# A fused attention and mixture kernel: w_in compacted in three spans of columns, and w2's last half summed in banks of its own

## The reference, cut to what matters

```python
attn_out = softmax(scale * q @ k.T + bias, causal window of 128) @ v        # 4 batches, 8 heads, 576 tokens, 64
x = attn_out as (2304, 512)

logits = x @ phi                                   # (2304, 32): 8 experts with 4 slots each
slot_input = softmax(logits, over tokens).T @ x    # (32, 512)
for e in range(8):                                 # w1[e]: 512 x 1024, w2[e]: 1024 x 512
    slot_out[e] = maximum(slot_input[e] @ w1[e], 0) @ w2[e]
c = softmax(logits, over slots)                    # (2304, 32)
x = c @ slot_out                                   # (2304, 512)

h = x @ w_in                                       # w_in: 512 x 2048
g = h * clip(h + 3, 0, 6) / 6
out = g @ w_out                                    # w_out: 2048 x 512
```

## Time and profile before

| | |
|---|---|
| median of 3 runs | 426.57 us (426.09 to 427.25) |
| the profiled execution | 426.3 us, span 424.5 us |
| TensorE matmuls busy | 415.3 us (98%) |
| VectorE busy | 234.5 us (55%) |
| ScalarE busy | 215.5 us (51%) |
| GpSimd busy | 70.6 us (17%) |
| DMA | 61.36 MB, mean 145 GB/s |

### The profile page before, as it was taken

One profiled execution on the slowest core, in us unless ns is written; L12 is line 12 of the kernel. 1 busy time (PEld: TensorE's weight loads), 2 busy tenths in 40 slices (PEclk: granted clock), 3 DMA queues, 4 the chain that ended last, 5 costly groups with the idle time before them and its releaser, 6 DMA issues.

```text
span 424.5 us, 9722 instructions
## 1 busy us (share of the span) xinstructions
PE 415.3 (98%) x3466; PEld 335.9 (79%) x3466; DVE 234.5 (55%) x701; ACT 215.5 (51%) x610; POOL 70.6 (17%) x112
## 2 busy tenths in 40 slices
PE   8799999999999999999999999999999999999996
PEld 7688788888878887635788888888888888888885
DVE  5568786777778777212745344444535344454532
ACT  4878777878678730002974434343443434343441
POOL 2233133223213310200792000000000000000000
PEclk9999999999999999999999999999999999999999
DMA  9958999898699469999901001010101001010101
GB/s 176 263 153 251 243 240 243 252 248 239 202 237 259 142 225 380 386 387 403 383 22 49 1 2 49 0 49 0 49 0 49 0 0 49 0 49 0 49 0 49
DMA packets 75587, 61.36 MB, mean 145 GB/s; under 512 B 57888, under 2 KB 57888, under 8 KB 75552
## 3 DMA queue, kind: packets, MB, share of 16 engines
q1 hardware_dynamic: 73456, 60.37, 47.2%
q10 hardware_dynamic: 2096, 0.52, 0.7%
HBM read 56.16 MB, written 4.72 MB: 143 GB/s over the span
## 4 chain that ended last, share of the span: by engine, by line
PE 87%; DVE 4%; DMA 3%; ACT 3%; issue 1%; SPq 0%; POOL 0%; POOLq 0%
PE probs_turned L1171 24%; PE out_turned L1171 23%; PE scores L921 7%; PE probs_turned L930 5%; PE scores L1157 4%; PE out_turned L946 4%; DMA weight_ring<-in_moe_w_dram 3%; PE scores L1094 3%; PE out_turned L950 3%; PE routes L979 3%; PE turns L961 2%; ACT probs L474 2%; PE turns L900 2%; PE turns L890 1%; DVE scores L620 1%
## 5 line engine op out<-in xcount | busy, mean ns | idle before, releaser
L833 DVE SCALAR_TENSOR_TENSOR g<-u,scores 128x512 f32<-128x512 f32 x71 | 48.9, 689 | 102.8 <-ACT u L533 102.7
L538 ACT ACTIVATE g_hi<-g 128x512 fp32r<-128x512 f32 x71 | 44.9, 632 | 113.6 <-PE out_turned L1171 113.5
L474 ACT ACTIVATE probs<-probs,rowmin 128x128 f32<-128x128 f32 (+1 forms) x160 | 62.0, 391 | 3.3 <-DVE rowmin L630 3.1
L1171 PE MATMUL probs_turned<-w_out_hi,g_hi 128*128 128x512 f32 x144 | 57.2, 397 | 0.1
L1171 PE MATMUL probs_turned<-w_out_hi,g_lo 128*128 128x512 f32 x144 | 56.1, 390 | 0.0
L1171 PE MATMUL out_turned<-w_out_hi,g_lo 128*128 128x512 f32 x144 | 56.1, 389 | 0.0
L1171 PE MATMUL out_turned<-w_out_hi,g_hi 128*128 128x512 f32 x144 | 56.0, 389 | 0.0
L1171 PE MATMUL probs_turned<-w_out_lo,g_hi 128*128 128x512 f32 x144 | 55.5, 395 | 0.0
L1171 PE MATMUL out_turned<-w_out_lo,g_hi 128*128 128x512 f32 x144 | 54.7, 389 | 0.0
L839 DVE TENSOR_TENSOR g_lo<-g,g_hi 128x512 fp32r<-128x512 f32 x71 | 51.1, 720 | 4.4 <-ACT g_hi L538 4.4
L533 ACT ACTIVATE u<-scores 128x512 f32<-128x512 f32 x71 | 41.3, 582 | 0.9 <-PE scores L1157 0.9
(11 more groups left out here) (164 smaller groups left out, 649.8 us busy)
## 6 DMA issues: line engine op xcount, KB each, us to landing
weight_ring<-in_moe_w_dram SPq DMA_DIRECT2D x30, 1024.0 KB, 8.1
out_dram<-y SPq DMA_DIRECT2D x18, 256.0 KB, 2.0
v_in<-in_v_dram SPq DMA_DIRECT2D x16, 256.0 KB, 3.9
weight_ring<-in_moe_w_in_dram SPq DMA_DIRECT2D x8, 512.0 KB, 13.1
weight_ring<-in_moe_w_out_dram SPq DMA_DIRECT2D x8, 512.0 KB, 13.6
q_in<-in_q_dram SPq DMA_DIRECT2D x15, 256.0 KB, 4.6
k_in<-in_k_dram SPq DMA_DIRECT2D x14, 256.0 KB, 4.5
weight_extra<-in_moe_w_dram SPq DMA_DIRECT2D x2, 1024.0 KB, 9.8
```

The source lines that it names most:

```text
L474: act.activation(probs[0:R, m % 2, h, :], probs[0:R, m % 2, h, :], ACT.Exp, bias=rowmin[0:R, m % 2, h:h + 1], scale=-1.0, accum_out=rsum[0 ...
L538: act.activation(g_hi[:, p % 2, :], g_sb[:, p % 4, :], ACT.Copy).then_inc(ghi_ready, 1)
L833: dve.scalar_tensor_tensor(out=g_sb[:, p % 4, :], in0=u_sb[:, p % 2, :], scalar=6.0, in1=bank[p % 4], op0=ALU.min, op1=ALU.mult).then_inc( ...
L1171: return pe.matmul(bank[4 + kk][:, :], g[:, p % 2, i * CHUNK + kk * P:i * CHUNK + (kk + 1) * P], w[:, c, :], start=(p == 0 and i == 0 and ...
```

## The change

It has three parts.

1. w2's last half (expert 7) goes to banks 0 and 1, 256 columns each, with a semaphore count for each. The other 15 halves are complete in bank 2 before it; VectorE copies them to a new tile `slot_out_main` and adds each bank to it while writing `slot_out`. Of the transposes, `turn_combine(0)` alone stands before the turning of slot_out, `turn_combine(1)` behind it, `turn_combine(2)` behind compact(0).
2. w_in is loaded and compacted in three spans of columns, 0 to 511, 512 to 1023 and 1024 to 2047. The loads stand among w_out's: w_in(0), w_out(0, 0), w_in(1), w_out(0, 1), w_in(2), then the rest of w_out. For the two quarters `compact` moves 128 columns per matmul and `spread_wp(0)` and `(1)` have four blocks of 128 columns with two matmuls each.
3. The orders of chunk 0 are new. On TensorE compact(1) goes ahead of projection (0,0), spread_wp(1) to between (0,0) and (0,1), compact(2) ahead of (2,0), spread_wp(2) and (3) between (2,0) and (2,1), and hidden 2 and 3, 4 and 5 behind projections (0,1) and (2,1). The dummy matmuls there go. On ScalarE and VectorE the copies and splits are moved to fit.

```diff
-            dve.wait_ge(ring_used, 2 * E)
+            dve.wait_ge(so_main_done, 1)
+            dve.tensor_copy(so_main[:, :], bank[2]).then_inc(so_main_copied, 1)
+            dve.wait_ge(so_main_copied, 1)
             for i in range(2):
-                dve.tensor_copy(so[:, i * CHUNK:(i + 1) * CHUNK], bank[2][:, i * CHUNK:(i + 1) * CHUNK])                   .then_inc(so_copied, 1)
+                half = slice(i * CHUNK, (i + 1) * CHUNK)
+                dve.wait_ge(so_last_done, i + 1)
+                dve.tensor_tensor(so[:, half], bank[i][:, 0:CHUNK], so_main[:, half], ALU.add).then_inc(so_added, 1)
...
+        SPANS = ((0, DFF // 4), (DFF // 4, DFF // 2), (DFF // 2, DFF))
...
             load_w_in(0)
-            load_w_out(0)
+            load_w_out(0, 0)
             load_w_in(1)
-            load_w_out(1)
-            load_w_out(2)
-            load_w_out(3)
+            load_w_out(0, 1)
+            load_w_in(2)
+            for n in range(1, PARTS):
+                for i in range(2):
+                    load_w_out(n, i)
...
             first_group()
             relu(1, 1)
-            copy_wp(1)
+            copy_combine(3)
             split_high(1)
-            copy_combine(3)
             for n in range(1, FPAIRS):
                 if n == 3:
                     copy_wp(3)
                 high(n, n)
+                if n == 1:
+                    copy_wp(1)
+                    copy_combine(4)
                 relu(n + 1, (n + 1) % FPAIRS)
-                if n == 1:
-                    copy_combine(4)
-                for p in {1: (2,), 2: (3, 4)}.get(n, (n + 2,)):
+                for p in {1: (), 2: (2, 3)}.get(n, (n + 1,)):
                     if p < FPAIRS:
                         split_high(p)
...
             first_group()
+            split_compact(1)
             gate(1, 1)
             for n in range(1, FPAIRS):
-                if n == 2:
-                    split_compact(1)
...
                 if n not in (1, 3):
                     low(n, n)
+                if n == 2:
+                    split_compact(2)
...
+            pe.wait_ge(*landed_of(PIECES - 1, 1))
+            for half in range(2):
+                for j in range(QUADS):
+                    ins = pe.matmul(bank[half][SLOTS * j:SLOTS * (j + 1), 0:CHUNK], hid_view[:, E - 1, QUADS + j, :],
+                                    w[:, QUADS + j, half * CHUNK:(half + 1) * CHUNK], start=True, stop=True,
+                                    tile_position=(0, SLOTS * j))
+                ins.then_inc(so_last_done, 1)
             turn_combine(0)
-            turn_combine(1)
...
             compact(0)
-            pe.wait_ge(comb_copied, 3)
-            turn_combine(3)
+            turn_combine(2)
             pe.wait_ge(picked, 1)
             pe.wait_ge(late_zeroed, 4)
             spread_wp(0)
-            spread_wp(1)
-            occupy(1, bank[0])
+            pe.wait_ge(comb_copied, 2)
             hidden(0, 0, 0)
             hidden(1, 0, 1)
+            pe.wait_ge(comb_copied, 3)
+            turn_combine(3)
+            compact(1)
             turn_combine(4)
-            occupy(3, bank[4])
 
 
             for p in range(FPAIRS):
-                if p == 1:
-                    pe.wait_ge(comb_copied, 4)
-                    compact(1)
+                if p == 2:
+                    pe.wait_ge(comb_copied, FILLS)
+                    compact(2)
                 if p >= 4:
                     hidden(p + 2, (p + 2) // FPAIRS, (p + 2) % FPAIRS)
                 project_rows(p, 0, p, 0)
                 if p == 0:
-                    hidden(2, 0, 2)
-                    hidden(3, 0, 3)
-                if p == 1:
-                    pe.wait_ge(comb_copied, FILLS)
+                    spread_wp(1)
+                if p == 2:
                     spread_wp(2)
                     spread_wp(3)
-                if p == 2:
-                    hidden(4, 0, 4)
-                    hidden(5, 0, 5)
                 project_rows(p, 0, p, 1)
+                if p in (0, 2):
+                    hidden(p + 2, 0, p + 2)
+                    hidden(p + 3, 0, p + 3)
```

More of the change, by code:

```diff
@@ L107, in layer_program @@
     so = place("slot_out", [P, D], tail + 14336)
+    so_main = place("slot_out_main", [P, D], early + 16384)
     hid = place("hid", [P, CHUNK], tail + 27392)
@@ L141, in layer_program @@
         ring_in = [[sem(f"ring_in{i}_{half}") for half in range(2)] for i in range(RING + 1)]
[L142 removed]
+        win_in = [sem(f"w_in_in{n}") for n in range(3 * KC)]
         wout_in = [sem(f"w_out_in{n}") for n in range(2 * PARTS)]
@@ L328, in load_piece, with load_w_in, load_w_out @@
                     load_half(n, i)
-            def load_w_in(r):
+            def load_w_in(u):
+                first, last = SPANS[u]
+                r = first // WHALF
                 sp.wait_ge(ring_used, WIN_SLOT + r + 1)
                 for c in range(KC):
-                    sp.dma_start(win_sb[r][:, c, :], w_in[c * P:(c + 1) * P, r * WHALF:(r + 1) * WHALF])\
-                      .then_inc(win_in[KC * r + c], 16)
-            def load_w_out(n):
+                    sp.dma_start(win_sb[r][:, c, first - r * WHALF:last - r * WHALF],
+                                 w_in[c * P:(c + 1) * P, first:last]).then_inc(win_in[KC * u + c], 16)
+            def load_w_out(n, i):
                 sp.wait_ge(ring_used, WOUT_SLOT + n // 2 + 1)
[L338 to L342, removed]
+                first = n * WROWS + i * WROWS // 2
+                sp.dma_start(wout_sb[n][:, i * WROWS // 2:(i + 1) * WROWS // 2, :],
+                             w_out[first * P:(first + WROWS // 2) * P, :].rearrange("(c p) n -> p c n", p=P))\
+                  .then_inc(wout_in[2 * n + i], 16)
             load_qk(0)
@@ L799, in _, with split_compact @@
                .then_inc(so_ready, 1)
[L801 to L807, removed]
+            def split_compact(u):
+                span = slice(SPANS[u][0] // QUADS, SPANS[u][1] // QUADS)
+                src = compact_bank(u)[:, 0:span.stop - span.start]
+                dve.wait_ge(wc_done, u + 1)
+                dve.tensor_copy(wc[:, 0, span], src).then_inc(wc_ready, 1)
+                dve.wait_ge(wc_ready, 2 * u + 1)
+                dve.tensor_sub(wc[:, 1, span], src, wc[:, 0, span].bitcast(f32)).then_inc(wc_ready, 1)
             def copy_wp_first(j):
@@ L1109, in _ @@
                 _, w = piece(E + n)
-                for i in range(2):
+                halves = 2 if n < E - 1 else 1
+                for i in range(halves):
                     pe.wait_ge(*landed_of(E + n, i))
@@ L1124, in _, with span_width, compact @@
             ins.then_inc(so_turned, 1)
-            turn_combine(2)
+            turn_combine(1)
             pe.wait_ge(so_ready, 1)
-            def compact(r):
+            def span_width(u):
+                return (SPANS[u][1] - SPANS[u][0]) // QUADS
+            def compact(u):
+                width, first = span_width(u), SPANS[u][0]
+                r = first // WHALF
                 for c in range(KC):
-                    pe.wait_ge(win_in[KC * r + c], 16)
+                    pe.wait_ge(win_in[KC * u + c], 16)
@@ L1135, in compact, with spread_block @@
                                         stop=(c == KC - 1), tile_position=(0, SLOTS * j))
                 ins.then_inc(wc_done, 1)
-            def spread_wp(n):
[L1139 to L1148, removed]
+            def spread_block(u, j, dst):
+                for i in range(2):
+                    pe.wait_ge(wc_ready, 2 * u + i + 1)
+                    ins = pe.matmul(dst, pick[:, j, 2 - 2 * i:6 - 2 * i, :].rearrange("p a s -> p (a s)"),
+                                    wc[:, i, SPANS[u][0] // QUADS:SPANS[u][1] // QUADS],
+                                    start=(i == 0), stop=(i == 1))
+                return ins
@@ new lines, in spread_wp @@
+            def spread_wp(n):
+                if n < 2:
+                    for j in range(QUADS):
+                        ins = spread_block(n, j, wp_first(j // 2)[:, j % 2 * P:(j % 2 + 1) * P] if n == 0 else
+                                           wp_bank(n)[:, j * P:(j + 1) * P])
+                        if n == 0 and j == 1:
+                            ins.then_inc(wp_done, 1)
+                else:
+                    for j in range(2):
+                        ins = spread_block(2, 2 * (n % 2) + j, wp_bank(n)[:, j * CHUNK:(j + 1) * CHUNK])
+                ins.then_inc(wp_done, 1)
```

23 lines of the change are left out of this document (15 added, 8 removed).

## The result

The changed kernel takes 427.70 us (median of 13 runs, 427.29 to 428.56) against a median of 426.07 us of 13 runs before. The ratio is 1.0036, 95% interval 1.0028 to 1.0045: 1.5 us slower (1.2 to 1.9), where 1.4 was forecast; the two medians are 1.6 us apart. One run of the kernel before took 1716.89 us and does not count in the ratio. The profiled execution took 427.29 us with a span of 425.6 us.

The account below looks back on a forecast made before the run. TensorE was taken to carry the chain from 193.60 us on. A front gain of 0.94 us against 2.3 us more ahead of hidden(4) put projection (4,0) 1.4 us later: 428.0 us, range 426.4 to 429.8.

Parts of the forecast that it names:

- slot_out and compact(0): Start of the front: slot_out is finished when TensorE reaches it, and compact(0) starts 0.7 us earlier, without waiting for w_in.
- Spread at weight-load price: spread_wp of a quarter: 0.117 us for each 128-column matmul, so 0.94 us per quarter in place of 0.47.
- columns alone: Rival on the quarter spreads: 0.06 us per matmul, 0.94 us less, 427.0 us, no change; chance 0.14.
- the f32 price: Rival on the quarter spreads: 0.22 us per matmul, 1.6 us more ahead of hidden(4), 429.6 us; chance 0.22.
- Front: TensorE's path to the first projection: it starts at 202.7 us against 203.64, a gain of 0.94 us.
- The balance: Front gains 0.94 us, but spread_wp(1) (0.94) and projection (2,1) (1.39) now precede hidden(4), which comes 1.4 us later.
- The chain's length: From hidden(4) through ScalarE and VectorE to projection (4,0): 4.81 us, unchanged from before.
- The cover of 4.78: TensorE's work between hidden(4) and projection (4,0) before the change: 4.78 us; 3.42 us after it.
- The wait: TensorE idles 1.4 us in sum before projections (3,0) and (4,0), until VectorE's g_lo is ready.
- GpSimd contends less now, which gives 0.2 for low(4): On VectorE, low(4) (0.88 us) could gain 0.2 us, since gate(5) of the same size takes 0.69.
- the wait does not appear: Rival at projection (4,0): hidden(4) to (4,0) takes under 3.42 us, TensorE runs through, 426.6 us; chance 0.10.
- Dummy matmuls: The dropped 8 instructions of 0.11 us lay in the break before the first projection; real work takes their place.

Follow-up runs that it names:

- e5: The kernel before with the slot_out part alone, w_in still in halves: 427.18 us, ratio 1.0012.
- e6: The changed kernel without the slot_out part: 428.62 us, ratio 1.0037.
- e4: The changed kernel with each 128-column matmul of the two quarter spreads cut in two of 64 columns: 429.63 us, ratio 1.0070.
- e7: The kernel of e2 with turn_combine(3) moved ahead of hidden(0): 426.16 us, ratio 0.9992.
- e3: The kernel before with only hidden(4) and (5) moved behind projection (2,1), no work added: 428.02 us, ratio 1.0026.
- e2: The changed kernel with compact(2), the spreads of wp's second half and hidden(4) and (5) back at their earlier places: 426.17 us, ratio 0.9998.
- e1: The changed kernel with low(4) ahead of gate(5) on VectorE, TensorE's program unchanged: 427.94 us, ratio 1.0034.
- e8: The kernel of e1 with GpSimd writing zeros to w_out_lo's last 8 blocks instead of subtracting: 426.71 us, ratio 1.0000.
- e9: The kernel of e2 without the slot_out part: 427.27 us, ratio 1.0018.
- e11: The kernel of e6 once more, on one chip with the changed kernel: 428.86 us, ratio 1.0052.

## Why the prediction was right, point by point

Behind w2's landing, in us:

| step | before | predicted | measured |
|---|---|---|---|
| compact(0) starts | 3.90 | 3.18 | 3.20 |
| compact of a quarter takes | - | 0.99 | 1.01 |
| spread of a quarter takes | - | 0.94 | 0.84 |
| projection (0,0) | 10.08 | 9.14 | 9.34 |
| hidden(4) | 20.74 | 22.11 | 22.41 |
| hidden(4) to (4,0) | 4.81 | 4.81 | 4.63 |
| projection (4,0) | 25.55 | 26.92 | 27.04 |

- *slot_out and compact(0)*: right to 0.02 us, cover included. w_in's quarter did not gate it. e5 and e6 show that the slot_out part and the quarter pay only together: with one of them alone the first projection starts 10.71 or 10.04 us behind w2, where it was 10.08.
- *Spread at weight-load price*: right in kind, 0.105 for 0.117 in size. e4 excludes the rival "columns alone", and the changed trace the f32 price. By the 81 ns of the Trainium skill (TensorE: Matmul & The Clock Gate, Back-to-back issue gap) the two would have been 1.30 us, an estimate; the first took 0.91 in e7's chain, the second 0.84, 1.75 in sum. The measurement decides: 0.105 us or more for each of these matmuls.
- *Front*: +0.94 forecast, 0.74 measured. The step mis-sized is the two hidden groups, which start 6.10 us behind w2 (6.04 forecast) and take 0.86 us, not 0.7, so that they end at 6.96 and not 6.74. They wait for VectorE's copies of wp, 0.43 us for the first where 0.38 was forecast.
- *The balance*: right. Two pieces more ahead of hidden(4), its chain uncovered: e3 gives this step alone 1.22 us at (4,0), e2 takes the loss away.
- *The chain's length*: misread, with luck. The 4.81 us were TensorE's own time in the kernel before: g_lo(4) had ended at 218.89, so the chain was 4.63 us with the 0.04 to the next start. (The cover of 4.78 is 4.81 too, with the 1.39 of its row for (2,1).) The changed kernel also has 4.63, since high(4) starts 0.14 us earlier and g_lo(4) takes 0.14 us longer.
- *The wait*: 1.4 forecast. Before (3,0) and (4,0) the weight loads stand idle for 0.28 and 1.02 us, the matmuls for 0.08 and 0.82, and restarting costs them the rest of 4.63 - 3.42 = 1.2 us. Another 0.15 us fall before (2,0), which I had not seen: g_lo(2) took 1.80 us beside GpSimd, 1.03 before.
- *Misses that offset each other*: at (4,0), 1.49 us measured for 1.37 forecast is 0.20 too much gain at the front and 0.10 too little on the way to hidden(4), less the 0.18 of the chain. That the total is this close is partly luck; the steps are right without it.
- *Where it was wrong*: "GpSimd contends less now, which gives 0.2 for low(4)". g_lo(4) took 1.02 us, more than the 0.88 before, and not 0.69; g_lo(0), both halves, took 1.49 for 0.76 before. In e1 that contention gave back the whole gain of a shorter chain. For the rival "the wait does not appear" the chain would have to be under 3.42 us; even with g_lo(4) at 0.69 it would be 4.3, and it took low(4) ahead of gate(5) as well as GpSimd out of the way (e8) to have no wait at (4,0) and (5,0).
- *Dummy matmuls*: dropping them cost the changed kernel no clock; its granted clock stayed at 1.00 in all its runs. e9 shows the risk (below).

## What to carry to other kernels

When a producer is moved behind a long piece of the bound engine, compare two numbers: the length of its chain through the other engines, and the bound engine's work that is left in between. Here 4.6 us met 3.4 us, and that comparison gave the sign and nearly the size, while the gain of 0.74 us at the front was real and went into the spread of 0.84 us that had moved behind it. Read such a length from the end of the last instruction of the chain, not from the start of the engine that may have come later. Before a chain is shortened at one link, look at what GpSimd reads beside that link: in e1 the wait only moved a group down. And a finer split of an operand did not pay where each matmul loads 128 weight columns (0.105 us with 128 columns moved, 0.117 with 256), and did with 32 weight columns.

## What the runs showed of the hardware

- A g_lo instruction of 128x512, two SBUF inputs, takes 0.68 us alone and up to 1.83 us beside GpSimd's w_lo (e1); beside a memset of GpSimd it takes 0.68 us.
- A matmul with a fresh load of 128 weight columns starts every 0.105 us with 128 columns moved and every 0.107 us with 64. Column-tiled ones with 32 weight columns follow their columns: 32 instructions take 1.01 us with 128, 1.86 with 256.
- In e9's profile the granted clock fell to 0.50, the 1.2 GHz level, while TensorE was working, after a stretch in which it was busy 2.36 of 3.00 us and one in which it was busy 1.47 of 1.50:

```profile
198.00:201.00 3.00, 2.36 (x42) 1.86 (x41) 1.10 (x4) 1.58 (x3) 1.70 (x2) 1.00 1.05 393
201.00:202.50 1.50, 1.47 (x8) 1.05 (x8) 0.99 (x3) 0.86 (x3) 0.81 (x1) 0.97 1.06 419
202.50:203.50 1.00, 1.00 (x21) 0.91 (x24) 0.85 (x3) 1.00 (x4) 0.00 (x0) 0.50 1.00 397
```

A quarter's compact took 1.87 us there instead of 1.01, and turn_combine(4) 1.13 instead of 0.68, 1.3 us in sum. e6 had the same 0.7 us of waits in the same place (busy 2.33 of 3.00) and kept its clock at 1.00 in its profile. So that profile of e9 can't be compared with e2's by its positions as they stand: projection (4,0) is 27.83 us behind w2, where 26.4 was forecast, and 26.5 without the 1.3. The spread of e9's runs goes with it: the three with a mean granted clock of 0.996 took 428.78 to 429.29 us, the nine with 1.00 took 426.43 to 427.51. In e11 one run of seven had 0.994 and took 431.23 us, the others at most 429.03. The kernels that keep the slot_out part, also without these dummy matmuls, had no run under 0.998. The kernel before has dummy matmuls at waits of this kind; that they prevent the fall is not shown.
